# q and k of fourteen head pairs loaded in 1024-byte packets, turned with a step of four tokens, and their misplaced quarters moved by transfers inside SBUF

## The reference, cut to what matters

```python
# q, k, v: (4, 8, 768, 64) float32
k_chunks = k.reshape(B, H, nc, 32, D)                    # 24 chunks of 32 keys
k_min, k_max = k_chunks.min(axis=3), k_chunks.max(axis=3)
ub = sum over D of max(q * k_min, q * k_max)             # an upper bound for each query and chunk
ub = where(causal by chunk, ub, -1e9)
sel = the 6 chunks of largest ub, of each query
scores = where(sel and causal, q @ k.T / 8, -1e9)
attn = softmax(scores);  x = attn @ v                    # (4, 8, 768, 64) -> rows (3072, 512)
```

## Time and profile before

| what | value |
|---|---|
| median of three runs | 299.71 us |
| the profiled execution, its own time | 297.4 us |
| its span, first to last instruction | 295.6 us |
| PE busy | 258.6 us (88%) |
| DVE busy | 195.4 us (66%) |
| ACT busy | 140.0 us (47%) |
| POOL busy | 123.0 us (42%) |
| mean granted clock of PE | 0.960 |
| DMA packets | 147124, of which 133151 are under 512 bytes |

### The profile page before, as it was taken

The page is one execution under the profiler, slowest core; times in us unless marked ns, Lnnn a source line. Parts: engine busy times, 40 slices in busy tenths (PEclk is TensorE's granted clock), DMA queues, the critical chain, the costliest instruction groups (busy, mean ns, idle before and its releaser), DMA issues.

```text
span 295.6 us, 12054 instructions
## 1 busy us (share of the span) xinstructions
PE 258.6 (88%) x5350; PEld 186.6 (63%) x5351; DVE 195.4 (66%) x549; ACT 140.0 (47%) x200; POOL 123.0 (42%) x241
## 2 busy tenths in 40 slices
PE   7799898989599899979798989899998999239994
PEld 7376758485485667756556767657666766137763
DVE  6868748374933979575839795899499569143432
ACT  2376373817319282727292727273837364402320
POOL 5032554625305261816160718171516141722882
PEclk9999999979779999999999999999999999757999
DMA  9989999999989999899999889999895044660483
GB/s 149 174 118 146 183 311 191 148 297 158 190 169 183 219 149 186 133 173 171 238 189 158 145 138 151 172 233 252 174 322 100 2 119 68 111 117 24 101 149 113
DMA packets 147124, 48.20 MB, mean 163 GB/s; under 512 B 133151, under 2 KB 137366, under 8 KB 147008
## 3 DMA queue, kind: packets, MB, share of 16 engines
q1 hardware_dynamic: 133280, 28.39, 47.4%
q0 software_dynamic: 10656, 18.65, 36.3%
q10 hardware_dynamic: 3136, 0.39, 0.9%
HBM read 56.69 MB, written 11.01 MB: 229 GB/s over the span
## 4 chain that ended last, share of the span: by engine, by line
PE 68%; DMA 12%; DVE 8%; issue 5%; ACT 4%; POOL 1%; ACTq 1%; SPq 0%; DVEq 0%; POOLq 0%
PE OB L617 24%; PE SC L557 19%; PE SC L576 4%; DMA vn<-in_v_dram 4%; DMA w2s<-in_moe_w_dram 4%; PE OB L1370 4%; PE SC L1344 3%; ACT EXB L585 3%; PE SC L488 3%; DMA qn<-x_rows,idx 2%; PE MM L672 2%; PE MM L557 2%; DMA qn<-in_q_dram 1%; PE MM L527 1%; PE OB L939 1%
## 5 line engine op out<-in xcount | busy, mean ns | idle before, releaser
L617 PE MATMUL OB<-vn,EXB 128*64 128x65 f32 x2520 | 83.8, 228 | 14.5 <-issue 9.5
L617 PEld LDWEIGHTS OB<-vn,EXB 128*64 128x64 f32 x2520 | 80.2, 144 | 20.5 <-issue 13.6
L585 ACT ACTIVATE EXB<-SC 128x1024 f32<-128x1024 f32 (+1 forms) x81 | 81.1, 1009 | 20.1 <-PE SC L576 14.3
L557 PE MATMUL SC<-qT,kT 64*128 64x512 f32 (+3 forms) x452 | 88.5, 480 | 0.6 <-ACT EXB L585 0.3
L557 PEld LDWEIGHTS SC<-qT,kT 64*128 64x128 f32 x452 | 37.6, 187 | 22.4 <-ACT EXB L585 10.4
L529 ACT ACTIVATE unsT<-MM 128x640 bf16<-128x640 bf16 x15 | 10.6, 704 | 81.7 <-PE MM L527 81.7
L594 POOL TENSOR_SCALAR_AFFINE_SELECT EXB<-EXB 128x256 f32<-128x256 f32 x94 | 38.0, 425 | 16.9 <-ACT EXB L585 16.5
L658 POOL CAST xp<-ES 128x768 bf16<-128x768 f32 x15 | 12.4, 825 | 57.9 <-DVE ES L656 40.2
L576 PE MATMUL SC<-unsT,ind 64*128 64x256 bf16 (+5 forms) x226 | 34.5, 299 | 0.7
L472 POOL TENSOR_TENSOR kmm<-kmx,kmm 128x24 f32<-128x24 f32 x14 | 5.4, 384 | 59.0 <-DVE kmx L471 59.0
L455 DVE STREAM_TRANSPOSE qT<-qn 128x768 f32<-128x768 f32 x16 | 15.6, 976 | 20.8 <-PE SC L576 18.5
(11 more groups left out here) (275 smaller groups left out, 344.7 us busy)
## 6 DMA issues: line engine op xcount, KB each, us to landing
w1s<-in_moe_w_dram POOLq DMA_DIRECT2D x32, 256.0 KB, 6.3
w2s<-in_moe_w_dram POOLq DMA_DIRECT2D x28, 256.0 KB, 6.2
vn<-in_v_dram SPq DMA_DIRECT2D x32, 192.0 KB, 6.1
kn<-in_k_dram SPq DMA_DIRECT2D x62, 96.0 KB, 3.2
qn<-in_q_dram SPq DMA_DIRECT2D x62, 96.0 KB, 5.7
out_dram<-w1s SPq DMA_DIRECT2D x2, 1536.0 KB, 11.5
out_dram<-out_dram SPq DMA_DIRECT2D x2, 1536.0 KB, 9.6
x_rows<-xp SPq DMA_DIRECT2D x3, 768.0 KB, 9.6
```

Source lines behind the costliest of these rows:

```text
L557: op("pe", lambda: pe.matmul(o, kT[j][pr, ts(kt)], qT[j][pr, q0:q1], start=not flags and (not cols or cols[0] == 0), stop=bool(flags)), r= ...
L585: op("act", lambda: ac.activation(Ex(st, None, 0, W), src, ACTF.Exp, scale=SCALE), r=pk, w=[f"E{st}"])
L617: op("pe", lambda: pe.matmul(OB[u * 64:u * 64 + 64, o:o + D + 1], Ex(st, h, c + u * 64, 64), vn[s][:, kt, h, :], start=first and h == 0, s ...
```

## The change

Pairs 0 and 1 are left as they were. For pairs 2 to 15 (`wide`):

- Each quarter transfer of q and k now reads runs of 256 floats, 1024 bytes: four whole tokens of 64 features. It has 96 such runs (32 partitions by 3) in place of 768. A quarter is now a head and one half of its tokens.
- `take_wide` replaces the transpose: two transposes on DVE per tensor, one for each half of the features, each 128 partitions by 384, reading 32 floats out of every 64 and writing with a step of four tokens. They write into a scratch buffer `T`, which lies in the back part of `w1s[6]`. There the quarters with half of the tokens or features exchanged lie on the wrong partitions.
- POOL then copies all of `T` into `qT` (or `kT`), which puts the right quarters in place, and SP issues four transfers from SBUF to SBUF, each 32 partitions by 384 floats (48 KB, runs of 1536 bytes), which write the other four quarters over it.
- `op` learns of parts: who reads `qT0` also reads its four parts `qT0m0` to `qT0m3`, the keys that the four transfers write. The transfers themselves name `qT` or `kT` among what they read.
- The two reductions of k and the difference on POOL are called one iteration later, behind the first two score steps (`take_k(i + 1, 1)`); `take_r` is called behind the fourth.
- The weights of expert 6's `w1`, whose place the scratch buffer uses, are loaded in iteration 14 in place of 13, the first of them after the readers of the scratch buffer.

```diff
--- before.py
+++ after.py
@@ -39,6 +39,7 @@
         self.snaps = {}
         self.lw = {}
         self.lr = {}
+        self.parts = {}
         for key in self.COMPUTE:
             self.sem(key)
 
@@ -70,6 +71,7 @@
                     clock[k2] = v2
 
     def op(self, ekey, fn, r=(), w=(), dsem=None, inc=True):
+        r = [p for k in r for p in [k] + self.parts.get(k, [])]
         is_dma = ekey in self.dma
         stream = self.stream.get(ekey, ekey)
         semkey = dsem if is_dma else ekey
@@ -349,11 +351,44 @@
                 def iv(off, rows, *dims):
                     return bass.AP(G, off, [[2 * S, rows]] + [list(d) for d in dims]).bitcast(I32)
 
+                HS = S // 2
+
+                def wide(i):
+                    return i > 1
+
+                def half_turned(j):
+                    return bass.AP(w1s[E - 2], 2 * Dm + j * 2 * S, [[DB * Fd, 128], [1, 2 * S]]).bitcast(F32)
+
+                for j in range(2):
+                    for n in "qk":
+                        sy.parts[f"{n}T{j}"] = [f"{n}T{j}m{x}" for x in range(4)]
+
+                def take_wide(i, n):
+                    j, s = i % 2, i % NB
+                    src, dst, T = (qn, qT, half_turned(0)) if n == "q" else (kn, kT, half_turned(1))
+                    row = T.ap[0][0]
+                    for x in range(2):
+                        a = bass.AP(src[s], x * 32, [[2 * NT * D, 128], [D, S * 2 // D // 2], [1, 32]])
+                        o = bass.AP(T.tensor, T.offset + x * HS, [[row, 128], [128, NT // 2], [1, 4], [4, 32]])
+                        op("dve", lambda: ve.transpose(o, a), r=[f"{n}n{s}{g}" for g in range(4)], w=[f"T{n}"] if x == 0 else [f"T{n}x"])
+                    op("gp", lambda: gp.tensor_copy(dst[j][:], T), r=[f"T{n}", f"T{n}x"], w=[f"{n}T{j}"])
+                    for x in range(4):
+                        h, u = x // 2, x % 2
+                        a = bass.AP(T.tensor, T.offset + (h * 64 + u * 32) * row + (1 - u) * HS, [[row, 32], [1, HS]])
+                        o = dst[j][h * 64 + (1 - u) * 32:h * 64 + (1 - u) * 32 + 32, u * HS:(u + 1) * HS]
+                        op("sp", lambda: sp.dma_start(o, a), r=[f"T{n}", f"T{n}x", f"{n}T{j}"], w=[f"{n}T{j}m{x}"], dsem=f"d_m{n}{j}")
+
                 def load(i, what="qkv", eng="sp", gs=range(4)):
                     b, p, s = i // NPB, i % NPB, i % NB
                     base = (b * H + 2 * p) * S * D
                     for nm, src, dst in (("qn", q, qn), ("kn", k, kn), ("vn", v, vn)):
                         if nm[0] not in what:
+                            continue
+                        if nm != "vn" and wide(i):
+                            for g in gs:
+                                a = bass.AP(src.tensor, src.offset + base + g * HS * D, [[4 * D, 32], [128 * D, NT // 2], [1, 4 * D]])
+                                o = bass.AP(dst[s], g * 32 * 2 * NT * D, [[2 * NT * D, 32], [4 * D, NT // 2], [1, 4 * D]])
+                                op(eng, lambda: sy.queue[eng].dma_start(o, a), w=[f"{nm}{s}{g}"], dsem=f"d_{nm}{s}{g}")
                             continue
                         if nm != "vn":
                             for g in gs:
@@ -417,7 +452,7 @@
 
                 def wload(e, part, after=(), js=range(4)):
                     for j in js:
-                        key = [f"w{part + 1}_{e}" if j == 0 else f"w{part + 1}_{e}{j}"] + (["LGA"] if part and e == E - 2 else [])
+                        key = [f"w{part + 1}_{e}" if j == 0 else f"w{part + 1}_{e}{j}"] + (["LGA"] if part and e == E - 2 else ["Tq", "Tqx", "Tk", "Tkx"] if e == E - 2 and j == 0 else [])
                         if part == 0:
                             src = bass.AP(moe_w1.tensor, moe_w1.offset + e * Dm * Fd + j * 128 * Fd, [[Fd, 128], [1, Fd]])
                             dst = w1s[e][:, j, :]
@@ -431,8 +466,8 @@
 
                 def wparts(i, n):
                     for m in {0: (0,), 1: (1,), 2: (2, 3)}[n]:
-                        if 0 < i < NP - 2:
-                            w = (i - 1) * 4 + m
+                        if 0 < i < NP - 3 or i == NP - 2:
+                            w = (min(i, NP - 3) - 1) * 4 + m
                             wload(w // 8, w // 4 % 2, (), (w % 4,))
 
 
@@ -452,6 +487,9 @@
 
                 def take_q(i):
                     j, s = i % 2, i % NB
+                    if wide(i):
+                        take_wide(i, "q")
+                        return
                     op("dve", lambda: ve.transpose(qT[j][:], qn[s][:].rearrange("p a b c -> p (a b c)")),
                        r=[f"qn{s}{g}" for g in range(4)], w=[f"qT{j}"])
 
@@ -461,9 +499,13 @@
                 def take_k(i, part=None):
                     j, s = i % 2, i % NB
                     kv = bass.AP(kT[j], 0, [[S, 128], [CHUNK, NCH], [1, CHUNK]])
-                    if part != 1:
+                    if wide(i) and part == 0:
+                        take_wide(i, "k")
+                        return
+                    if part != 1 and not wide(i):
                         op("dve", lambda: ve.transpose(kT[j][:], kn[s][:].rearrange("p a b c -> p (a b c)")),
                            r=[f"kn{s}{g}" for g in range(4)], w=[f"kT{j}"])
+                    if part != 1 or wide(i):
                         op("dve", lambda: ve.tensor_reduce(kmm[j][:, 0, 0:NCH], kv, AX, ALU.min), r=[f"kT{j}"], w=[f"kmm{j}"])
                     if part == 0:
                         return
@@ -1141,10 +1183,12 @@
                     if live and kk == 1:
                         rank_pred()
                         rank_cmp(bb, 5, 4)
+                    if i and i + 1 < NP and wide(i + 1):
+                        take_k(i + 1, 1)
                     scores(i, 2 if i else 3, 4)
                     wparts(i, 2)
-                    if i == 0:
-                        take_r(1)
+                    if i + 1 < NP:
+                        take_r(i + 1)
                     if live and kk == 2:
                         rank_count(bb)
                         rank_slot(bb)
@@ -1179,11 +1223,10 @@
                             logits_take(i - 1)
                     if i + 2 < NP:
                         take_q(i + 2)
-                        take_r(i + 2)
                     if i + 1 < NP:
                         bounds_out(i + 1)
                     if i + 2 < NP:
-                        take_k(i + 2)
+                        take_k(i + 2, 0)
                     if i == 1:
                         tables()
                     if i == 3:
```

## The result

| kernel | median of its runs, us | time against before |
|---|---|---|
| before, run beside it (4 runs) | 299.16 | 1 |
| changed (4 runs, 458.50 to 463.64) | 460.86 | 1.541, interval 1.529 to 1.553 |

The changed kernel is slower, as forecast, but by 162 us and not by 89. The mechanism of the forecast is in the trace; its size is near the one that was given to the rival "the moves land late". A ratio compares the faster runs of both kernels, and the runs behind the traces of experiments 8 and 10 were over 1.5% slower than the fastest run of their kernel, so what is read from these two traces is an indication only.

The account below looks back on a forecast made before the run. The prediction took PE to bound the kernel, 14.8 us per pair, with transfers costing up to about 15 us. Its terms, 18.05 + 14 × 20.0 + 1 + 16 + 70.1, gave 385 us of span; it said 388, range 340 to 440.

Parts of the forecast that it names:

- The mechanism of the forecast: Moves into one tensor wait for each other's landings, POOL's next q copy for X; the turn, 20.0 us, bounds the loop.
- the moves land late: Rival: under the weights' and loads' traffic s goes to 2.7, 26.3 us per turn, about 480 us; chance 0.08.
- X: The end of the reduction of k's maximum for a pair, from which the forecast counted each turn.
- X to the first move, 4.95 us: POOL's work in order, 4.0 us, then the q copy, 0.85, and 0.1 to SP: first move issued at X + 4.95.
- The fixed part, 7.4 us: Per turn, all but the seven landings: 4.95 to the first move, 0.53 plain issue, 1.89 for k's two reductions.
- s: Step from one move's issue through its landing to the next; taken as 1.8 us, between 1.05 and 3.5, seven per turn.
- the terms "on top": First turn starts behind 16 loads on SP, 1 us; moves behind four big transfers on q1 wait, 16 us in all.
- the tail: Span behind 225.5 us, with a chain of weight landings the change leaves alone: 70.1 us.
- The four transfers of zeros, 4 us each: Four 1536 KB transfers (two fills, two copies) on q1 right ahead of moves: 4 us each, 16 in all, bounds 0 and 39.
- The half transposes: DVE's two for one cost between 0.77 and 1.94 us per tensor, hidden since DVE waits for the moves anyway.
- What it removes: 75,264 packets, at most 79 us of all 16 engines' time; at best waits of 5.0 + 9.5 us, and 2 for k.
- The range: 340 to 440 us, chance 0.80: s from 1.4 with few delays, 17.2 us per turn, to 2.3 with queueing, 23.5.

Follow-up runs that it names:

- experiments 8 and 10: 8: Experiment 1 with k's transposes called right behind q's, 321.3 us, 1.060; 10: kernel before with v's loads called ahead of q's and k's, 298.9 us, 1.010.
- Experiment 1: Changed kernel, but the four moves into one tensor don't wait for each other, only for POOL's copy: 323.8 us, 1.079 against before.
- experiment 5: Changed kernel with all 52 weight transfers of the loop issued behind it: 22.6 us per pair; total 477.4 us, of no use as weights come late.
- experiment 2: Kernel before with only the long-packet loads of q and k and the old single transposes, so data misplaced: 293.4 us, 0.977 against before.
- experiment 3: Changed kernel with the loop's loads of q, k and v issued on ACT's queue: 460.2 us (one run), 26.2 us per pair.
- experiment 9: Kernel before with v of the loop issued on ACT in place of SP: 303.3 us, 1.013 against before.

## Why the prediction was wrong, step by step

- **The mechanism: right.** Each move behind the first waits for a landing, POOL's copy waits for the X of the pair before, and the loop is bound by that turn. Experiment 1 takes 137 of 162 us away with that wait alone.
- **X to the first move, 4.95 us: right where the LGA sum stands in between** (4.80 to 4.82 us in six turns), too long elsewhere (2.6 to 4.3 us in seven, which have no LGA sum there). The forecast left out that the sum waits for the new bounds and logits of PE; it was luck that this way is only 0.14 us longer than POOL's own order. The copies took 0.82 us for q and 1.03 in the mean for k (0.85 forecast).
- **The fixed part, 7.4 us: nearly right** (7.3 in the turn shown, 7.0 in the mean of 14).
- **The size of s, 1.8 us: right for a move alone on the engines, wrong for seven in a turn. This is the step that failed.** The quiet landing is 1.82 to 1.87 us. But (26.1 − 7.4) / 7 = 2.7 us is the mean, which is also that of the 98 landings themselves, and that is the rival "the moves land late": s = 2.7, 26.3 us per turn, with a chance of 0.08. (Its total, some 480 us, is higher than the 461 measured mainly because the transfers of zeros are in the measured mean and stood beside it in the rival's sum.) The arguments against the rival were that a move has two packets per engine and that q1 is mostly drained when the moves are issued. The eight loads of q and k had indeed landed, but v's had not in any of the 13 turns behind the first, nor in 12 of them the weights, which POOL issues just ahead of the copy and which are not on q1 at all; without them s is 2.3 (experiment 5).
- **Where the 72 us of error lie** (457.1 − 385 of span): the first q moves of the 14 turns landed after 1.96, 9.63, 8.77, 3.99, 6.76, 4.60, 3.76, 4.38, 6.69, 5.06, 4.61, 3.55, 10.61 and 6.44 us, 80.8 in all against 14 × 1.8 + 17 = 42.2 with the terms "on top": 38.6. The four moves behind them that the forecast held at 1.8 (second and third of q, first and second of k) add some 33 more, the last two k moves, which were quiet, 1, and the tail took 73.7 us, not 70.1. The fixed parts were 5 us shorter in all than 14 × 7.4.
- **The four transfers of zeros, 4 us each: too small as well.** The moves behind them landed after 9.63, 8.77, 10.61 and 6.44 us, 28 us over a quiet move in place of 16. Some 12 of the 28 any first move met: the other nine behind the first turn took 4.8 us in the mean.
- **The half transposes: inside their bounds.** 128x384 with a step of four tokens took 0.87 us (q) and 0.88 (k), two for one 0.97 of the earlier trace rows.
- **What it removes: the bounds held.** The bound was 14.5 us for the two waits; experiment 2 got about 7, the wait for v with little else. Of the 79 us of all 16 engines that were the most the packets could free, 27 went.
- **The range** ended at 23.5 us per turn, on a mean landing of 2.3 with 20 us of queueing. It left out traffic in every turn, though the earlier trace rows showed a median of 3.2 us for a load under it, and that row was used as the upper end of s. Between ends of 1.05 and 3.5 the value was taken from the quietest load; the measured mean of 2.7 lies between what the two rows gave.

The Trainium skill's figure for a transfer (DMA: Bandwidth & Descriptors, "Anatomy of one DMA"), about 2.0 us fixed, is near the quiet landing of 1.85 us measured here, though the page gives it for GpSimd's transfers. The busy landings of 3.6 to 10.6 us above are no part of it.

What stays open: which transfer holds which move. The first moves of ordinary turns fell when weights went (2.9 us in the mean in experiment 5) and stayed near 4.4 when the loads changed queue; a run without the loads, or without those of v alone, wasn't tried. One thing more goes with late moves, which neither the forecast nor the experiments had in view. The page of experiment 5 has it as a queue of its own (packets, MB, share of 16 engines):

```profile
q8 instruction: 42, 0.69, 0.6%
```

These are packets of 16 KB, by the queue's name of the program's instructions, about 1 us each. In experiment 5, of the moves that landed with no other load, store or weight transfer under way, the 14 whose last stretch (from 1 us behind the issue to 0.35 us before the landing) met such a packet landed after 2.1 to 3.2 us, 2.8 in the mean; of the other 74, 71 landed within 1.95. This is a reading of one trace; how much of the changed kernel's 461 us it explains is not shown.

## What to carry to other kernels

A small transfer inside a serial chain costs its landing each time, and that landing is set by whatever else the DMA engines carry at that moment: read from the order what is issued in the few us ahead of it on every queue, and don't price it at the quietest landing of the trace; here that was 1.8 us, the median under traffic 3.2, and the chain's mean 2.7. Before adding such a chain to save packets, run the kernel with the saving alone; here it was worth 2.3%, and with the turning the kernel was 8% slower than before even when no move waited for another, 10% slower than with the saving alone. A key that a helper widens for readers also widens it for the writers that name it as read: look at what each wait of a new instruction names.

## What the runs showed of the hardware

- A transfer of 48 KB inside SBUF (32 partitions by 1536 bytes) lands 1.82 to 1.87 us after its issue when little else is under way, and 3.6 to 6.8 us where ten loads and two weight transfers were issued just ahead (the nine first moves of a turn without zeros). All moves of the changed kernel (least, median, most):

```profile
DMA to landing us min/median/max: 1.8/1.9/10.6
```

- Putting the loads on a different issuing engine didn't shield it (experiment 3, 26.2 us per pair against 26.1). An issue on ACT takes 0.37 to 1.52 us, 0.69 in the mean of 28, and stands on the path with 12 us in all, where the wait that it removes was 5.0 (experiment 9).
- A float32 copy of 128x768 on POOL takes 0.82 us, about the same as the cast to bf16 of the earlier trace rows; the k copies take 1.03 in the mean, why is not shown:

```profile
L374 POOL COPY kT<-w1s 128x768 f32<-128x768 f32 x14 | 14.4, 1027 | 39.1 <-DVE w1s L373 29.3 <-DVE rk L1023 4.3 <-DVE iota L476 3.3
...
L374 POOL COPY qT<-w1s 128x768 f32<-128x768 f32 x14 | 11.5, 824 | 2.8 <-DVE w1s L373 2.8
```

- A DVE transpose that reads 32 floats of every 64 and writes with a step of 16 bytes costs 0.87 us for 384 columns, nearly as much as 768 contiguous ones (0.97 in the earlier trace rows):

```profile
L373 DVE STREAM_TRANSPOSE w1s<-qn 128x384 f32<-128x384 f32 x28 | 22.1, 869 | 2.3 <-DMA qn<-in_q_dram 2.3
```
